# Attention, routed experts and a gated convolution on one core: the last transposes of prob and the last output tile as whole-array products, q and k tails turned later

## What is computed

```python
batch, n_heads, seq, head_dim = (4, 8, 576, 64)
...
scores = scale * np.matmul(q, k.transpose(0, 1, 3, 2))
causal = np.triu(np.ones((S, S), dtype=bool), k=1)
cum = np.cumsum(np.maximum(s, 0.0), axis=-1)
bias = -(cum[:, :, :, None] - cum[:, :, None, :])
scores = np.where(causal, -1e9, scores + np.minimum(bias, 0.0))
attn = np.exp(scores - np.max(scores, axis=-1, keepdims=True))
attn = attn / (np.sum(attn, axis=-1, keepdims=True) + 1e-09)
return np.matmul(attn, v)
```

## Time and profile before

| | |
|---|---|
| timed runs | 779.73, 779.76, 787.46 us; median 779.76 |
| profiled execution | 785.7 us, of which span 784.0 us |
| mean granted TensorE clock over the span | 0.971 |
| TensorE busy | 739.0 us (94% of the span), 4838 products |
| VectorE, GpSimd, ScalarE busy | 436.3, 335.0, 308.0 us |
| attention's last product begins | 211.15 us after the span's start |

### The profile page before, as it was taken

How to read it: one execution, slowest core, us unless ns; L and a number is a source line. 1 busy time by engine, 2 the same in 40 slices (tenths; PEclk the granted TensorE clock), 3 DMA queues, 4 the chain that set the end, 5 groups by cost and what they waited for, 6 DMA issues and landing times.

```text
span 784.0 us, 14869 instructions
## 1 busy us (share of the span) xinstructions
PE 739.0 (94%) x4838; PEld 614.9 (78%) x4838; DVE 436.3 (56%) x1034; ACT 308.0 (39%) x608; POOL 335.0 (43%) x442
## 2 busy tenths in 40 slices
PE   6999999999839998999999999999599999999998
PEld 4787777777627886888888888887399998989986
DVE  5777878778677433544445444453259746546420
ACT  4777787677420013111111311100058544535521
POOL 7668787887317359554444854400421100000000
PEclk9999999999958999999999999999699999999999
DMA  8888787774143773434343443100321110010011
GB/s 175 204 219 215 185 225 192 212 181 112 36 154 96 236 226 125 141 138 167 136 168 134 146 167 135 66 28 28 97 66 34 51 38 28 14 40 14 28 41 54
DMA packets 99703, 93.11 MB, mean 119 GB/s; under 512 B 62108, under 2 KB 71604, under 8 KB 99636
## 3 DMA queue, kind: packets, MB, share of 16 engines
q1 hardware_dynamic: 80196, 46.27, 21.9%
q10 hardware_dynamic: 15968, 34.67, 12.7%
q0 software_dynamic: 3472, 11.28, 4.9%
HBM read 76.13 MB, written 16.06 MB: 118 GB/s over the span
## 4 chain that ended last, share of the span: by engine, by line
PE 59%; DMA 5%; POOL 3%; DVE 2%; issue 2%; ACT 1%; ACTq 0%; POOLq 0%; SPq 0%; DVEq 0%
PE row_bank L1170 15%; PE wide_bank L1155 14%; PE row_bank L1356 13%; PE wide_bank L1345 12%; DMA x_slots<-x_rows,token_of 5%; POOL ring L870 2%; PE wide_bank L1181 2%; PE bank L1322 1%; PE bank L1136 1%; POOL x_slots L1070 1%; DMA y_tok<-y_sorted,place_i 0%; PE bank L962 0%; DVE x_tr L1377 0%; DMA y_sorted<-y_sb 0%; ACT x_tr L1429 0%
## 5 line engine op out<-in xcount | busy, mean ns | idle before, releaser
L870 POOL TENSOR_TENSOR ring<-raw_w,ring 128x2048 fp32r<-128x2048 f32 x30 | 137.5, 4605 | 87.2 <-ACT ring L860 87.2
L1155 PE MATMUL wide_bank<-ring,xs_tr 128*128 x600 | 146.4, 401 | 6.4 <-POOL ring L870 3.8
L1170 PE MATMUL row_bank<-ring,h_tr 128*128 x600 | 144.9, 397 | 1.9 <-DVE h_tr L1227 1.9
L860 ACT ACTIVATE ring<-raw_w 128x2048 fp32r<-128x2048 f32 x30 | 55.8, 1907 | 226.2 <-DMA raw_w<-in_moe_w_dram 196.6
L1155 PEld LDWEIGHTS wide_bank<-ring,xs_tr 128*128 128x128 f32 x600 | 113.5, 193 | 30.1 <-issue 7.3
L1170 PEld LDWEIGHTS row_bank<-ring,h_tr 128*128 128x128 f32 x600 | 112.0, 190 | 25.2 <-issue 2.1
L1345 PE MATMUL wide_bank<-x_tr,ring 128*128 128x288 f32 x768 | 108.4, 299 | 2.7 <-DVE x_tr L1377 2.7
L1345 PEld LDWEIGHTS wide_bank<-x_tr,ring 128*128 128x128 f32 x768 | 104.3, 190 | 3.9 <-DVE x_tr L1377 3.2
L1356 PE MATMUL row_bank<-ring,g_tr 128*128 128x512 f32 x432 | 100.2, 390 | 1.4 <-DVE g_tr L1384 1.4
L1356 PEld LDWEIGHTS row_bank<-ring,g_tr 128*128 128x128 f32 x432 | 80.4, 188 | 17.7 <-DVE g_tr L1384 1.6
L219 POOL TENSOR_SCALAR bias<-ncum_row,cum_col 128x128 f32<-128x128 f32 (+3 forms) x128 | 67.0, 532 | 48.8 <-DVE row_min L513 37.2
(11 more groups left out here) (191 smaller groups left out, 976.8 us busy)
## 6 DMA issues: line engine op xcount, KB each, us to landing
raw_w<-in_moe_w_dram ACTq DMA_DIRECT2D x12, 2048.0 KB, 9.9
ncum_row<-cum_rows SPq DMA_DIRECT2D x15, 512.0 KB, 4.2
y_sorted<-y_sb SPq DMA_DIRECT2D x25, 256.0 KB
raw_w<-in_moe_w_dram SPq DMA_DIRECT2D x12, 512.0 KB, 4.0
ncum_tail<-cum_rows SPq DMA_DIRECT2D x32, 144.0 KB, 4.4
out_dram<-out_sb ACTq DMA_DIRECT2D x18, 256.0 KB, 2.0
v_nat<-in_v_dram SPq DMA_DIRECT2D x32, 128.0 KB, 2.5
q_nat<-in_q_dram SPq DMA_DIRECT2D x30, 128.0 KB, 4.0
```

The lines of the kernel that those rows point to most:

```text
L860: nc.scalar.activation(high, whole, ACT.Copy).then_inc(high_ready, 1)
L870: nc.gpsimd.tensor_tensor(low, whole, high.bitcast(F32), ALU.subtract).then_inc(low_ready, 1)
L1155: last = nc.tensor.matmul(h_bank[:, half, :], xs_tr[:, a, kb, :], ring[:, bass.ds(n, 1), b, at:at + FH].rearrange("p a c -> p (a c)"), sta ...
L1170: last = nc.tensor.matmul(y_bank[:, :], h_tr[:, a, kb, :], ring[:, bass.ds(n, 1), 2 + b, kb * D:(kb + 1) * D].rearrange("p a c -> p (a c)" ...
```

## The change

The tail end of `prob` is turned by one whole-array transpose of its last 128 columns (448 to 575), of whose result the upper 64 partitions are used, as before; it now lies in columns 384 to 511 of its bank. `out_tr` gets 64 more columns, zeroed once at the start, and the tail's turned output becomes a product with a stationary operand of 128 columns. `turn_qk_tails(p+1)` goes from before `turn_prob_0(p)` to between `turn_prob_2(p)` and `turn_k(p+1)`, into the bank of unit 5, of which it uses the free columns 384 to 511; `move_qk_tails(p+1)` goes to between `move_second(p, 2)` and `move_k(p+1)`. The waits follow the banks.

```diff
-    out_tr = sb("out_tr", [P, S])
+    out_tr = sb("out_tr", [P, NT * P])
...
+        nc.gpsimd.memset(out_tr[:, S:NT * P], 0.0)
         nc.gpsimd.memset(tail_end_tr[:, :], 0.0).then_inc(zeros_ready, 1)
...
         def turn_qk_tails(p):
-            u, bank = p % 2, turn(p - 1, 2)
+            u, bank = p % 2, turn(p - 1, 7 if p else 2)
             nc.tensor.transpose(bank[:, 3 * P:4 * P], q_nat[u][:, FULL, :], identity[:, :]).then_inc(tails_turned, 1)
...
         def turn_prob_2(p):
-            pe.wait_ge(tails_moved, min(p + 2, PAIRS))
             above(pe, moved_by_dve, FULL * p)
...
-            nc.tensor.matmul(turn(p + 1, 2)[P - TAIL:P, 0:P], prob[unit(p, UNITS - 1) % 4][:, BODY:S], identity[:, :], start=True, stop=True)\
+            nc.tensor.transpose(turn(p + 1, 2)[:, 3 * P:4 * P], prob[unit(p, UNITS - 1) % 4][:, S - P:S], identity[:, :])\
                 .then_inc(tail_end_turned, 1)
...
         def turn_out(p):
...
             pe.wait_ge(moved_by_dve, FULL * (p + 1) + (2 if p + 1 < PAIRS else 0))
+            pe.wait_ge(tails_moved, min(p + 3, PAIRS))
...
         def turn_out_end(p):
+            if p == 0:
+                pe.wait_ge(zeros_ready, 1)
...
-            turned_and_gated(small_bank(p)[0:TAIL, 0:WIDE], p, BODY, S).then_inc(out_end_turned, 1)
+            turned_and_gated(small_bank(p)[:, 0:WIDE], p, BODY, NT * P).then_inc(out_end_turned, 1)
...
                 turn_tail_end(p - 1)
-            if more:
-                turn_qk_tails(p + 1)
             turn_prob_0(p)
...
             turn_prob_2(p)
             if more:
+                turn_qk_tails(p + 1)
                 turn_k(p + 1)
...
         def move_second(p, i):
             dve.wait_ge(prob_turned, unit(p, 2 * i + 1) + 1)
+            if i == 2 and p + 1 < PAIRS:
+                dve.wait_ge(tails_turned, p + 2)
...
         def small_written(p):
...
             dve.wait_ge(tail_end_turned, min(p + 2, PAIRS))
-            dve.wait_ge(tails_turned, min(p + 4, PAIRS))
...
                 scale_gates_end(p - 2)
-            if more:
-                move_qk_tails(p + 1)
             add_bias(p, 5)
...
             move_second(p, 2)
             if more:
+                move_qk_tails(p + 1)
                 move_k(p + 1)
```

More of the change, by code:

```diff
@@ L528, in move_tail_end @@
             above(dve, pv_done, NT * p)
-            nc.vector.tensor_copy(tail_end_tr[P - TAIL:P, :], turn(p + 1, 2)[P - TAIL:P, 0:P]).then_inc(moved_by_dve, 1)
+            nc.vector.tensor_copy(tail_end_tr[P - TAIL:P, :], turn(p + 1, 2)[P - TAIL:P, 3 * P:4 * P]).then_inc(moved_by_dve, 1)
         def move_qk_tails(p):
-            u = p % 2
+            u, bank = p % 2, turn(p - 1, 7 if p else 2)
             dve.wait_ge(tails_turned, p + 1)
-            nc.vector.tensor_tensor(q_tail[u][:, :, :], turn(p - 1, 2)[:, 3 * P:3 * P + TAIL].unsqueeze(1).to_broadcast([P, 2, TAIL]),
+            nc.vector.tensor_tensor(q_tail[u][:, :, :], bank[:, 3 * P:3 * P + TAIL].unsqueeze(1).to_broadcast([P, 2, TAIL]),
                                     own_head[:, :, :], ALU.mult)
-            nc.vector.tensor_copy(k_tr[u][:, BODY:S], turn(p - 1, 2)[:, 3 * P + TAIL:4 * P]).then_inc(tails_moved, 1)
+            nc.vector.tensor_copy(k_tr[u][:, BODY:S], bank[:, 3 * P + TAIL:4 * P]).then_inc(tails_moved, 1)
         def move_k(p):
```

## The result

Timed 21 times each, the changed kernel took 780.21 us in the median (775.75 to 786.26) and the kernel before 784.91 us (779.16 to 790.50). The ratio is 0.9947 with a 95% interval of 0.9923 to 0.9972: 0.53% faster, about 4.2 us. The profiled execution took 776.45 us with a span of 774.7 us, against 784.0 before; that 9.3 us is more than the change is worth, as the experiments show. (A span is the time from the first to the last instruction of a profile; the granted clock is the share of TensorE's full speed that it was given.)

A forecast was written before the change was run, and what follows sets the result against it. Attention was taken to be bound by TensorE's sequence, busy 20.00 of 20 us. Terms of 2.6 + 0.2 + 0.4 + 0.25 - 0.24 + 0.45 = 3.66, say 3.6 us, off the 779.76 median gave 776.2 us, range 774.2 to 782.3.

The forecast's parts named there:

- rival A: After attention's gain: VectorE or ScalarE is the next bound at once; 779.8 us, down to a gain of 1; chance 0.12.
- Steady pair: TensorE's stretch with the two padded products in pairs 2 to 14: 0.20 us gained each, bounds 0.03 and 0.20.
- the sum: All gains and losses of the change: 2.6 + 0.2 + 0.4 + 0.25 - 0.24 + 0.45 = 3.66, say 3.6 us.
- Pair 1: Stretch from the q transposes to the next scores, without turned output yet: 1.37 us to 0.97 counting 0.11 later, gain 0.4.
- Pairs with logits: Pairs 5, 9 and 13, where VectorE decides: gain 0.3, perhaps 0.4, instead of 0.2; 0.45 us more in all.
- Last group: Attention's last output group, ten passes over 1.65 us: 1.40 us after the change, gain 0.25.
- Pair 0: Before `qk(1, 0)`, where no V products cover the tails' moves: loss 0.24 us, between 0.1 and 0.44.
- the base: Whole-kernel starting time: median of the timed runs, 779.76 us, from which 3.6 us were taken to give 776.2.
- rival D: TensorE's granted clock: each fall or its absence worth 1.9 us; slower 782.1 us, chance 0.15, faster 774.3, chance 0.05.
- B: `move_k` too late for the next pair's `qk` in every pair: about 785.3 us, with half of it 782.5; chance 0.07.
- the cover of 0.45 us: Pair 8: `move_k` recorded to 118.12, TensorE at the next `qk` at 118.57, so 0.45 us left and no wait.
- C: Padded products lose the half-column passes' overlap: at 0.17 us a pass, 0.03 gained a pair, 778.4 us; chance 0.08.

The follow-up runs named there:

- 11 and 12: Low halves of experts 2 and 3 made between GpSimd's gathers, on the kernel before and on the changed one: 779.54 us (ratio 0.9932) and 776.00 us (0.9891).
- experiments 2 and 3: Changed kernel with the tail's turned output (2) or the tail end of `prob` (3) a half-column product again: steady pair 12.50 and 12.61 us against 12.21.
- experiment 1: Kernel before with only the q and k tails moved later, both half-column products kept: steady pair 12.39 to 12.40 us, pairs 5, 9 and 13 12.39.
- experiment 6: Changed kernel with pair 1's q and k tails at the old place in pair 0: units 2 and 3 transposes to `qk(1, 0)` 3.58 us, against 4.09.
- experiment 10: Changed kernel again, timed 12 times beside the one with both start repairs: 783.47 us, ratio to before 0.9983 (0.9944 to 1.0022).

## Why the prediction was right or wrong

**The change itself: right in mechanism and near in size.** 3.6 us were forecast. The ratio gives 4.2 (2.2 to 6.0), the comparison at equal clock 4.0, both with room for 3.6. Attention's last output group begins 2.7 us earlier in the first two profiles, 3.0 in the means of two profiles with the old attention (211.15, 211.30) and five with the new (207.60 to 208.57); 3.4 were forecast. That it passes to the end is shown by 11 and 12, where rival A, an absorbed gain, is out. So attention shows 3 us, short of the forecast, and the whole times 3.4 to 4.2; whether the last microsecond between 3 and 4 is real, the runs don't decide.

**Its terms.** Steady pair: forecast 0.20, measured 0.19. This was no luck: the sum took the old stretch as measured, 1.22 us, and the new one by the rates of whole-array rows, so it needed no price for the form or the sharing. It was when I split that gain for the experiments that I had the form wrong: 0.16 us, the price of one change, for the way in and back, which costs 0.29 (experiments 2 and 3), and nothing for the sharing, which is worth 0.22. Pair 1: forecast 0.4, of which 0.11 returns later, so 0.51 in its stretch; measured 0.52 (1.37 to 0.85 us). Pairs with logits: forecast 0.35 each, measured 0.50 to 0.51. I wrote "0.3, perhaps 0.4"; experiment 1 shows that VectorE's lateness, all of its 0.31 to 0.33, went by the move, and the pair's own 0.19 came on top. Last group: 0.14 instead of 0.25. Pair 0: I priced the loss at 0.24 "between 0.1 and 0.44"; it is 0.51 (experiment 6), since `move_second` came 0.17 later and not 0.1 earlier. Pair 2's bias load wasn't in the sum: a loss of 0.36 in the first profile, nothing in the second. All in all attention gives 3.1 us (3.0 to the start of the last group and 0.14 in it) where the sum had 3.66.

**What failed is what was said of the measurement: what it can tell from no change, and the base.** The prediction says "A measurement of this kernel tells about 1% (7.8 us) from no change" and so puts 0.94 on a result within that bound. No row stood behind the 1%. With 21 runs each the interval is a quarter of a per cent either way, 0.9923 to 0.9972; it leaves out no change. So the result lies within 7.8 us and is told from no change all the same: the 0.5% that the mechanism gave is seen as a gain. With 12 runs of the same kernel it was not seen (experiment 10), so that it showed at all depended on the number of runs.

The base failed too. "I take the same 3.6 us from the median: 776.2 us." The median of three, 779.76, lies near the lower end of a spread from 779 to 790 us; 21 runs have 784.91. So the changed kernel's median, 780.21, is 4.0 us above the 776.2, though inside the range of 774.2 to 782.3. The profile said so: its own execution stood 5.9 us above that median, and I explained this by falls of the clock alone (rival D). The step before the fall, TensorE's wait for the weights of expert 2, stood in the trace of before, 3.8 us long, and the forecast left it out.

**The rivals.** B did not occur: the cover of 0.45 us held with 0.4. C, sharing lost, was a real cost of 0.22 us a pair, but smaller than the form's 0.29; its padded passes at 0.17 did not occur, they stand 0.12 apart. A did not occur either. D, the clock, was given 5.9 us; two executions of the changed kernel lie 8 us apart, part of it by the clock and part by a wait that I had not priced. Two of its readings need setting right. Between the 24 products up to 544.92 us and those from 547.69 TensorE ran eight more products (L1181) and waited 1.91 us, not all of the 2.8. And behind that same wait the products take 5.71 us at full clock, so the fall is worth 1.6 us and not 1.9.

## What to carry to other kernels

A half-column product alone between whole-array ones cost 0.29 us for the form and saved no pass. Padding it was best here (12.21 us), two of them side by side second (12.39), one alone worst (12.50 and 12.61). Price a change of form by both of its parts, the pass before it and the pass after it, and count the way back. Before a forecast leans on a median of a few runs, look for the wait in the profile that could vary with DMA timing, and judge small changes by a stretch that repeats (here a pair to 0.01 us) or at equal granted clock. A repair at the start can be lost entirely in where a clock fall lands later.

## What the runs showed of the hardware

Going from whole-array to half-column products and back cost 0.29 us with one product between (experiments 2 and 3). Each of the two changes lengthened the step before it by 0.09 us and the step after it by some 0.05. With an extra product, and a turned-output product of 146 columns on the way back, it cost 0.34.

Two half-column products that write different halves of the partitions ran side by side: four passes in 0.39 us, as long as two alone.

Two executions of the same kernel differ enough in their gathers (the last at 282.75 or 287.89 us) to lengthen one wait of TensorE from 0 to 4.5 us. With the clock behind it, that gives times 8 us apart. The 24 products behind it took 5.7 to 5.8 us after a wait of up to 1.3 us and 7.1 to 8.6 after 2.8 to 4.5. Before the last expert's output products one and the same wait of 1.92 us was followed by 24 products in 5.71 us in one profile and in 7.30 in another, so the length of the wait alone did not decide.
